# A gated linear attention feeding a token mixer and a gated feed-forward: attention in chunks of 128 tokens instead of 64

## The reference, cut to what matters

```python
# attention: q, k, v, alpha are (4 batches, 8 heads, 768 tokens, 48)
for t in range(S):
    state = alpha[:, :, t, :, None] * state + einsum('bhd,bhe->bhde', k[:, :, t], v[:, :, t])
    y[:, :, t] = einsum('bhd,bhde->bhe', q[:, :, t], state)
# mixer: x is the attention's output, (4, 768, 384)
theta = x @ w_theta
y = einsum('ts,bsd->btd', w_tok_r, x * cos(theta)) + einsum('ts,bsd->btd', w_tok_i, x * sin(theta))
u = x + y
u = u + maximum(u @ w_ch, 0)
# feed-forward with a convolution of three taps over the tokens
h = maximum(u @ w_in, 0); gate = sigmoid(conv(h)); out = (h * gate) @ w_out
```

## Time and profile before

| | |
|---|---|
| median of three runs | 605.9 us |
| the profiled execution: its own time | 603.88 us |
| its span | 602.2 us |
| attention: first to last scan `after` | 6.7 to 125.1 us |
| last copy of the attention's output | 141.7 us |
| TensorE / VectorE / ScalarE / GpSimd busy over the span | 90% / 77% / 47% / 34% |
| HBM read / written | 37.53 MB / 14.16 MB |

### The profile page before, as it was taken

The page is one execution under the profiler, slowest core; times in us unless marked ns, Lnnn a source line. Parts: engine busy times, 40 slices in busy tenths (PEclk is TensorE's granted clock), DMA queues, the critical chain, the costliest instruction groups (busy, mean ns, idle before and its releaser), DMA issues.

```text
span 602.2 us, 14808 instructions
## 1 busy us (share of the span) xinstructions
PE 541.1 (90%) x5626; PEld 529.6 (88%) x5626; DVE 460.9 (77%) x669; ACT 280.1 (47%) x555; POOL 207.2 (34%) x178
## 2 busy tenths in 40 slices
PE   2777687766599999999999999999999999999996
PEld 2676677765599999999999999899999999999996
DVE  5999999991456575757666656669999899998984
ACT  3566655553334344333433444434555545554443
POOL 7545544540124112412141226313333333323332
PEclk9989987988799999999999999999999999999999
DMA  8988888835120022002100400130202202021011
GB/s 193 259 235 237 228 244 231 236 93 160 40 61 27 15 92 61 26 13 92 61 26 13 145 14 0 40 120 1 80 1 78 78 0 78 0 78 39 2 40 40
DMA packets 33922, 52.39 MB, mean 87 GB/s; under 512 B 3536, under 2 KB 23760, under 8 KB 33872
## 3 DMA queue, kind: packets, MB, share of 16 engines
q1 hardware_dynamic: 31472, 48.16, 28.1%
q10 hardware_dynamic: 2400, 3.54, 1.6%
HBM read 37.53 MB, written 14.16 MB: 86 GB/s over the span
## 4 chain that ended last, share of the span: by engine, by line
PE 55%; issue 13%; POOL 4%; DVE 2%; ACT 1%; POOLq 0%; ACTq 0%; DVEq 0%
PE y_bank L1059 19%; PE y_bank L1109 13%; PE theta_bank L1097 6%; PE x_bank L1097 6%; PE theta_bank L1049 6%; PE y_bank L1080 5%; POOL z L827 3%; PE x_bank L1040 1%; POOL z L806 1%; POOL mixing_w L820 0%; POOL in_w L799 0%; DVE turns L941 0%; ACT z L860 0%; DVE angle L951 0%; ACT L869 0%
## 5 line engine op out<-in xcount | busy, mean ns | idle before, releaser
L1059 PE MATMUL y_bank<-mixing_w,z 128*128 128x384 f32 x864 | 156.3, 337 | 1.9 <-POOL z L806 1.8
L1059 PEld LDWEIGHTS y_bank<-mixing_w,z 128*128 128x128 f32 x864 | 149.4, 188 | 3.2 <-POOL z L806 3.2
L827 POOL TENSOR_TENSOR z<-x_tokens,z 128x384 fp32r<-128x384 f32 x64 | 68.8, 1075 | 145.9 <-ACT z L910 129.0
L1109 PE MATMUL y_bank<-mixing_w,z 128*128 128x384 f32 x576 | 111.3, 337 | 2.7 <-POOL z L827 2.7
L806 POOL TENSOR_TENSOR z<-z_full,z 128x384 fp32r<-128x384 f32 x48 | 49.3, 1050 | 167.8 <-ACT z L860 167.8
L1109 PEld LDWEIGHTS y_bank<-mixing_w,z 128*128 128x128 f32 x576 | 101.7, 188 | 3.6 <-POOL z L827 2.3
L1017 DVE SCALAR_TENSOR_TENSOR z_full<-out_rows,taps,x_rows 128x384 f32<-128x384 f32 x64 | 79.1, 1237 | 2.2
L1097 PE MATMUL theta_bank<-mixing_w,in_w 128*128 128x386 f32 x288 | 55.7, 337 | 0.0
L1097 PE MATMUL x_bank<-mixing_w,in_w 128*128 128x386 f32 x288 | 55.7, 337 | 0.0
L1097 PEld LDWEIGHTS theta_bank<-mixing_w,in_w 128*128 128x128 f32 x288 | 50.9, 188 | 0.0
L1097 PEld LDWEIGHTS x_bank<-mixing_w,in_w 128*128 128x128 f32 x288 | 50.9, 188 | 0.0
(11 more groups left out here) (92 smaller groups left out, 824.9 us busy)
## 6 DMA issues: line engine op xcount, KB each, us to landing
a_in<-in_a_rows SPq DMA_DIRECT2D x32, 148.5 KB, 3.6
k_in<-in_k_rows SPq DMA_DIRECT2D x32, 144.0 KB, 3.3
q_in<-in_q_rows SPq DMA_DIRECT2D x32, 144.0 KB, 3.8
v_in<-in_v_tokens SPq DMA_DIRECT2D x16, 288.0 KB, 5.0
x_scratch<-x_rows SPq DMA_DIRECT2D x32, 144.0 KB, 3.4
x_in<-x_scratch SPq DMA_DIRECT2D x24, 192.0 KB, 2.6
y<-x_all SPq DMA_DIRECT2D x7, 576.0 KB, 3.3
u_scratch<-u_sum ACTq DMA_DIRECT2D x6, 576.0 KB, 3.6
```

Source lines behind the costliest of these rows:

```text
L827: pool.tensor_tensor(g[k % 4][1][:, :], gated[k % 2], g[k % 4][0][:, :].bitcast(F32), ALU.subtract).then_inc(g_low.sem, 1)
L1059: ins = pe.matmul(y_bank[2 * d + half][:, 0:HALF], z[s % 2][part][zp][:, d * P:(d + 1) * P], mixing_w[part][wp][:, s, half * HALF:(half + ...
L1109: ins = pe.matmul(out_bank[half][t][:, 0:MODEL], g[k % 4][gp][:, t * P:(t + 1) * P], out_w[wp][f], start=f == 0 and i == 0, stop=f == FF_T ...
```

## The change

What it does:

- `CHUNK` becomes 128: 6 chunks instead of 12. `PACKED` is 780 instead of 792. There are 12 score products of 128 x 128 per pair instead of 24 of 64 x 64, so that the mask covers 1536 instead of 768 numbers per partition; 5 carried states per head instead of 11.
- The output is made by halves of 384 tokens in one PSUM bank (`x_half`), each copied out before the next one begins (`copy_half`). The inside part has all 128 rows of the array and 48 columns, the states' part 64 rows and 48 columns, the scores 64 rows and 128 columns. Each half waits for its own inside part (`x_inside`) before the states are added.
- GpSimd scales q one step later (for pair p at the start of a step), after the previous pair's state scan is done (`stated.done(pool, p - 1)`).
- The low parts of the mixer's weights move from VectorE to GpSimd, at the end of its step.
- VectorE's mask moves behind the scan `before`; on the DMA queue q's load moves ahead of k's and is for pair p+2 after `q_done` of pair p; the wait for the constants moves from VectorE's start to its first mask; the check of magnitudes moves from the end of all steps into the last but one.

The diff, cut to its core. Of TensorE's part the new lines alone are shown; the old ones are L368 to L427 above.

```diff
-CHUNK = 64
+CHUNK = P
 CHUNKS = SEQ // CHUNK
 SPAN = CHUNK + 2
-COUPLES = CHUNKS // 2
 PACKED = CHUNKS * SPAN
+ENTERED = CHUNKS - 1
...
-        turned = ctx.enter_context(nc.psum_tensor("turned", [P, 2, 512], F32))
-        weighed = ctx.enter_context(nc.psum_tensor("weighed", [P, 2, 512], F32))
-        x_sum = ctx.enter_context(nc.psum_tensor("x_sum", [P, 2, 512], F32))
+        turned = ctx.enter_context(nc.psum_tensor("turned", [P, 1024], F32))
+        weighed = ctx.enter_context(nc.psum_tensor("weighed", [P, 2, CHUNKS, CHUNK], F32))
+        x_sum = ctx.enter_context(nc.psum_tensor("x_sum", [P, 512], F32))
+        added = turned[:, SEQ:SEQ + ENTERED * HEAD_DIM]
...
+                if p is not None and p + 2 < PAIRS:
+                    q_done.done(sp, p)
+                    rows(q_in, q_rows, got_q, p + 2)
...
-                if i is not None and i + 2 < PAIRS:
-                    q_done.done(sp, i)
-                    rows(q_in, q_rows, got_q, i + 2)
                 if o is not None:
-                    x_copied.done(sp, o)
+                    x_copied.done(sp, 2 * o + 1)
...
+                if p is not None:
+                    stated.done(pool, p - 1)
+                    got_q[p % 2].done(pool, p // 2)
+                    x_made.done(pool, 2 * (p - 3) + 1)
+                    before_done.done(pool, p)
+                    pool.tensor_tensor(chunked(q_scaled[p % 3][:, :]), chunked(q_in[p % 2][:, :]), packed(before[p % 2][:, :], 1),
+                                       ALU.mult).then_inc(q_done.sem, 1)
                 if i is not None:
                     after_done.done(pool, i)
                     got_k[i % 2].done(pool, i // 2)
                     scored.done(pool, i - 2)
                     pool.tensor_tensor(chunked(k_scaled[i % 2][:, :]), chunked(k_in[i % 2][:, :]), packed(after[i % 2][:, :], 2),
                                        ALU.mult).then_inc(k_done.sem, 1)
-                    before_done.done(pool, i)
-                    got_q[i % 2].done(pool, i // 2)
-                    x_made.done(pool, i - 3)
-                    pool.tensor_tensor(chunked(q_scaled[i % 3][:, :]), chunked(q_in[i % 2][:, :]), packed(before[i % 2][:, :], 1),
-                                       ALU.mult).then_inc(q_done.sem, 1)
+                if 0 <= piece < len(pieces):
+                    piece_high.done(pool, piece)
+                    pool.tensor_tensor(pieces[piece].low, pieces[piece].raw_of(raw[piece % 2]), pieces[piece].high.bitcast(F32),
+                                       ALU.subtract).then_inc(piece_low.sem, 1)
...
-                    act.activation(k_tokens[p % 2][:, :, :].rearrange("p (h j) d -> p h (j d)", h=2), turned[:, :, 0:HALF],
+                    act.activation(k_tokens[p % 2][:, :, :].rearrange("p c d -> p (c d)"), turned[:, 0:SEQ],
                                    ACT.Copy).then_inc(k_copied.sem, 1)
+                if o is not None:
+                    copy_half(o, 0)
...
                 if p is not None:
                     kv_made.done(act, p)
                     stated.done(act, p - 2)
-                    act.activation(state_in[p % 2][:, :, :].rearrange("p e (j h) -> p e j h", h=2),
-                                   turned[:, :, 0:COUPLES * HEAD_DIM].rearrange("p h (j e) -> p e j h", e=HEAD_DIM),
+                    act.activation(state_in[p % 2][:, :, 0:ENTERED], added.rearrange("p (c e) -> p e c", e=HEAD_DIM),
                                    ACT.Copy).then_inc(state_fed.sem, 1)
-                if o is not None:
-                    x_made.done(act, o)
-                    stored[o % 2].before(act, o // 2, 1)
-                    act.activation(x_rows[o % 2][:, :].rearrange("p (j h t) -> p h j t", h=2, t=CHUNK),
-                                   x_sum[:, :, 0:HALF].rearrange("p h (j t) -> p h j t", t=CHUNK), ACT.Copy).then_inc(x_copied.sem, 1)
                 if i is not None:
                     before_done.done(act, i)
                     measured.done(act, i - 1)
                     act.activation(magnitudes[:, :], before[i % 2][:, :], ACT.Abs, accum_out=sums[:, i:i + 1]).then_inc(measured.sem, 1)
+                if o is not None:
+                    copy_half(o, 1)
                 if i is None and p is not None:
                     act.activation(carried.unused[:, :], ident[:, 0:1], ACT.Sin)
 
+            def copy_half(o, half):
+                x_made.done(act, 2 * o + half)
+                if half == 0:
+                    stored[o % 2].before(act, o // 2, 1)
+                act.activation(x_rows[o % 2][:, half * HALF:(half + 1) * HALF], x_sum[:, 0:HALF], ACT.Copy).then_inc(x_copied.sem, 1)
+
+            act.wait_ge(const, N_CONST)
+            act.wait_ge(dve_const, N_DVE_CONST)
...
-                if p is not None:
-                    scored.done(dve, p)
-                    x_made.done(dve, p - 2)
-                    dve.tensor_tensor(scores[p % 2][:, :, :, :], weighed[:, :, 0:HALF].rearrange("p g (j t) -> p g j t", t=CHUNK),
-                                      causal[:, :].rearrange("p (g j t) -> p g j t", g=1, j=1).broadcast_to([P, 2, COUPLES, CHUNK]),
-                                      ALU.mult).then_inc(masked.sem, 1)
-                if i is not None:
                     inverted.done(dve, i)
                     q_done.done(dve, i - 2)
                     measured.done(dve, i - 2)
                     dve.tensor_tensor_scan(before[i % 2][:, :], a_in[i % 2][:, :], resets[:, 0:PACKED],
                                            1.0, ALU.mult, ALU.add).then_inc(before_done.sem, 1)
-                if 0 <= piece < len(pieces):
-                    piece_high.done(dve, piece)
-                    dve.tensor_tensor(pieces[piece].low, pieces[piece].raw_of(raw[piece % 2]), pieces[piece].high.bitcast(F32),
-                                      ALU.subtract).then_inc(piece_low.sem, 1)
                 if p is not None:
+                    dve.wait_ge(const, N_CONST)
+                    scored.done(dve, p)
+                    x_made.done(dve, 2 * (p - 2) + 1)
+                    dve.tensor_tensor(scores[p % 2][:, :, :, :], weighed[:, :, :, :],
+                                      causal[:, :].rearrange("p (g c t) -> p g c t", g=1, c=1).broadcast_to([P, 2, CHUNKS, CHUNK]),
+                                      ALU.mult).then_inc(masked.sem, 1)
...
+            def x_half(o, half):
+
+                chunks = range(half * CHUNKS // 2, (half + 1) * CHUNKS // 2)
+                masked.done(pe, o)
+                x_copied.done(pe, 2 * o + half - 1)
+                got_v[o % 3].done(pe, o // 3)
+                for c in chunks:
                     for g in range(2):
+                        ins = pe.matmul(x_sum[head(g), tokens(c - chunks[0])], v_in[o % 3][:, c, g, :], scores[o % 2][:, g, c, :],
+                                        start=c == chunks[0], stop=c == 0, skip_group_check=True)
+                ins.then_inc(x_inside.sem, 1)
+                stated.done(pe, o)
+                x_inside.done(pe, 2 * o + half)
+                for c in chunks:
+                    for g in range(2):
                         if c:
+                            ins = pe.matmul(x_sum[head(g), tokens(c - chunks[0])], state[o % 2][half_of(g), :, c - 1],
+                                            q_scaled[o % 3][half_of(g), tokens(c)], start=False, stop=True, skip_group_check=True)
+                ins.then_inc(x_made.sem, 1)
 
             def step(i, p, o, piece):
                 if p is not None:
                     k_done.done(pe, p)
                     state_fed.done(pe, p - 1)
+                    for c in range(CHUNKS):
+                        ins = pe.transpose(turned[:, tokens(c)], k_scaled[p % 2][:, tokens(c)], ident[:, :])
                     ins.then_inc(k_back.sem, 1)
                 if o is not None:
+                    x_half(o, 0)
                 if p is not None:
                     k_copied.done(pe, p)
                     got_v[p % 3].done(pe, p // 3)
+                    for c in range(ENTERED):
+                        for g in range(2):
+                            ins = pe.matmul(added[half_of(g), c * HEAD_DIM:(c + 1) * HEAD_DIM], k_tokens[p % 2][:, c, half_of(g)],
+                                            v_in[p % 3][:, c, g, :], start=True, stop=True)
                     ins.then_inc(kv_made.sem, 1)
+                    q_done.done(pe, p)
+                    masked.done(pe, p - 1)
+                    for c in range(CHUNKS):
+                        for g in range(2):
+
+                            if c == 4 and g == 0:
+                                scored_four.done(pe, p)
+                            ins = pe.matmul(weighed[:, g, c, :], k_scaled[p % 2][half_of(g), tokens(c)], q_scaled[p % 3][half_of(g), tokens(c)],
+                                            start=True, stop=True)
+                            if c == 1 and g == 1:
```

(3 more changed lines are left out.)

106 lines of the change are left out of this document (33 added, 73 removed).

## The result

Median 582.98 us (4 runs, 581.54 to 583.93) against 605.92 (4 runs, 604.88 to 606.45): a ratio of 0.962 [0.960, 0.965], 22.9 us less.

What follows compares the result with a forecast made beforehand. The DMA queue was to bound attention's step at 7.1 us: 16 + 13 x 7.1 = 108.3, taken as 109, plus 17.9 gives 127 instead of 142.5, so 603.9 - 15.5 = 588.4, about 590 as median; range 583 to 601.

Steps and rivals of the forecast that it cites:

- VectorE's step: Attention, VectorE's work per step: two scans, reciprocal, mask and state scan sum to 6.2 us, where the old rows gave 8.5.
- The end from the last `after` to the last copy: End of attention: 17.9 us instead of 17.4, as the output goes half by half through one bank.
- the DMA is the new bound: Attention's steps: the DMA queue at 7.1 us sets the step, above VectorE's 6.2 and TensorE's 6.7; chance 0.50.
- the floor of 7.1 us: Attention, DMA queue: 1.87 MB per step at 264 GB/s takes at least 7.1 us.
- the other end, 276 GB/s: Attention, DMA queue: if only the share counts, 237/0.86 = 276 GB/s, a floor of 6.7 us a step.
- TensorE at 6.7: Attention, TensorE's step: 5.4 streamed, 0.6 for two waits, 0.7 for shape changes: 6.7 us, range 6.0 to 7.4.
- five changes of shape: Attention, TensorE: five further changes of array shape a step cost 0 to 0.27 us each, half taken.
- Rival D: Attention, TensorE: scores and states don't overlap in pairs, 9.3 us a step, 12 slower, 618 us; chance 0.10.
- The larger chunk gives TensorE nothing: Attention, TensorE: its groups take 5.4 us per step with chunks of 128, as before.
- the allowance: Attention, last `after`: 109 us taken instead of 108.3, for waits added by two close limits, 6.7 and 7.1.
- Rival B: Attention, DMA queue: it delivers what is asked, 6.2 to 6.7 us a step, 580 us; chance 0.10.
- The sign that the prediction named for its own failure: Attention, VectorE: gaps ahead of the mask that end with TensorE's scores; also a share below 0.9 or state scan above 1 us.

Runs made afterwards that it cites:

- the run of the chunk alone: The kernel after with low parts back on VectorE and q scaled at its old place without the wait for the state scan: 588.47 us, ratio 0.973.
- asked for more: The kernel after with v of every pair loaded a second time into a tile that nothing reads: 592.33 us, ratio 0.978.
- everything but the chunk: The kernel before, at chunks of 64, with the change's q place, q load place, low parts and order of VectorE and TensorE: 599.73 us, ratio 0.993.
- with less to load: The kernel after with k and q loaded for their first 128 tokens only from the third pair on: 582.63 us, ratio 0.962.
- the run with the added products: The kernel after with 16 unused products of the identity at TensorE's end of attention: 584.45 us, ratio 0.968.

## Why the prediction was right and wrong

**Right**: the direction and its main reason. VectorE's step is the sum that was worked out: 1.75, 0.20, 1.78, 1.76, 0.75 against 1.75, 0.2, 1.76, 1.75, 0.73. The state scan stands free of GpSimd's products in nearly all steps (median 0.748; once 1.45, early, and once 2.38, at the end). Part of the reason is another than the one given: by the run of the chunk alone it is free of the q product without q's wait for it. GpSimd's products take 1.69, the low part 1.82 (forecast 1.7, at worst 2.3). The end from the last `after` to the last copy is 18.9 (forecast 17.9). What follows attention moved by 0.5 us.

**Wrong, the step "the DMA is the new bound"**: the floor of 7.1 us took the 264 GB/s of one stretch as what the queue can do. It gives 283 in the same kernel later and 293 when asked for more. The stretch from 18 to 32 us had a share of 1.01 and moved 264 in the kernel before and 267 at 1.05 in the one after; both are early stretches, so they were no measure of the steady one. By 293 GB/s the floor is 6.4. The forecast had the other end, 276 GB/s from "if only the share counts", and even that was too low (1.87/0.276 is 6.8 us, where the prediction writes 6.7). This step makes most of the miss: 13 steps of 6.63 instead of 7.1 are 6.1 of the 7.0 us, and they put the time 0.02 us below the range. TensorE's chain of 6.55 us is what bounds the step in its place.

**Right by size, but taken for second**: TensorE at 6.7 (6.0 to 7.4) is 6.55 and sets the step. Its terms: scores 0.122 a round of two, inside 0.118, states 0.126, new states 0.062: 0.72 + 1.42 + 1.46 + 1.26 + 0.62 = 5.48 (forecast 5.4). The two waits inside are 0.32 each, start of inside to start of states 1.03 less 6 rounds of 0.118 (forecast 0.6 for both). What is left, 6.55 - 5.48 - 0.64 = 0.43, is five changes of shape at 0.09 (forecast 0.7; the full run-out, 1.35). The records' own starts say the same: inside the transposes they are 0.109 us apart, and from the last one to the next group's first it is 0.203. The rule of the Trainium skill cited there (TensorEngine Tiling (Array Packing), Key Properties), that a change of tiling mode drains TensorE, had been priced at 0.27 a change; the trace shows a third of that, so a full run-out is not paid. Rival D did not come: in the states' part two corners of the array write one bank, on different partitions, at 0.126 us a round for two records, where a transpose alone streams its 128 columns in 0.12, so they overlap; the scores overlap in pairs as well, 0.122 a round. The sentence of the Trainium skill that spoke for D (the same page, Gotcha 1) does not hold for two such corners here.

**Wrong, the step "The larger chunk gives TensorE nothing"**: true of the streamed time (5.4 and 5.48), false of the engine. The runs split the 22.9 us: everything but the chunk 5.3, the chunk alone 16.4; together 21.7. At chunks of 64 TensorE stops for 1 to 2.5 us in most steps once VectorE no longer hides it, 22 us in all, and each time goes on some 1.5 us after a packet of instructions has landed; with 94 records a step it is 0.9 us in all. The sign of it was in the earlier trace rows and was passed over, since I read groups by their mean and not their idle time by its releaser. With the chunk left out my sum would have given 590 as well (VectorE 8.5 - 1.5 - 0.9 = 6.1 us, below the queue's 7.1), 10 us less than was measured.

**The total**: in the profiled execution, last `after` 104.2 instead of 109: 13 steps of 6.63 instead of 7.1 are 6.1 less, the start 2.0 more (step 2 at 18.0, not 16), 0.7 of the allowance not needed. Last copy 123.1 instead of 127, the rest 0.5 less: 583.9 instead of 588.4. The other 2.6 us of the 7.0 are the distances of the medians from their profiled executions: 2.0 added for before, of which rounding to 590 took 0.4, and 1.0 by which the one of after lies above its median. Rival B's number, 6.2 to 6.7 a step and 580, came nearest, with a chance of 0.10: the queue does deliver, but TensorE and not the queue sets what it is asked for. The sign that the prediction named for its own failure, gaps ahead of the mask that end with TensorE's scores, is what the profile shows.

**Open**: why the instruction packets come too late, and what of it is the number of records and what the DMA load; the two longer steps of the profile after (one has a 0.55 us stop of this kind in its transposes, one 0.33 in its states; with less to load there are none, but neither are there in the run with the added products, whose loads are whole), and why the part behind attention varies by 3 us (459.0 to 462.0), which the stretches of half clock do not settle.

## What to carry to other kernels

Before an engine is called free, read its idle time by its releaser, also where another engine hides it: a stop inside a group with no releaser comes into the open as soon as the cover goes, and fewer, larger instructions can be worth more than the streamed time says. A rate that a queue showed at full share is a lower bound and belongs to the mix of that stretch; take it from the steady stretch or test it with a load that nothing reads. When three engines stand within 0.5 us of each other, removing one wait moves the step by no more than the next one's distance.
